# Weighting the values with full-width TensorE blocks instead of two 64-column halves

## The reference

```
scores = where(causal, -1e9, (q @ k.T) / sqrt(D));  scores -= scores.max(-1)
a      = exp(scores);  a /= a.sum(-1) + 1e-9
local  = a @ v
phi(x) = where(x > 0, x, exp(x) - 1) + 1
mem    = (phi(q) @ M_prev) / (phi(q) @ z_prev + 1e-6)
out    = g * mem + (1 - g) * local,   g = sigmoid(beta)
x      = out laid out as (B*S, H*D)
x      = (s * relu(x @ w_in)**2 + b) @ w_out                  # first layer
x      = layernorm(h * softmax(h)) * g_ln @ w_out2, h = x @ w_in2   # second
```

## Time and profile before

| | |
|---|---|
| median of 3 runs | 835.33 us |
| profiled execution | 835.52 us, span 833.5 us |
| PE, PEld busy | 98%, 86% of the span |
| DVE, ACT, POOL busy | 62%, 41%, 41% |
| L662 PE passes, 128 x 64 stationary, 65 moving columns | 1600, 70.9 us busy, mean 226 ns |
| L662 weight loads | 1600, 61.7 us busy, mean 137 ns |
| granted clock of TensorE (mean) | 0.999 |

### The profile page before, as it was taken

The page is one execution under the profiler, slowest core; times in us unless marked ns, Lnnn a source line. Parts: engine busy times, 40 slices in busy tenths (PEclk is TensorE's granted clock), DMA queues, the critical chain, the costliest instruction groups (busy, mean ns, idle before and its releaser), DMA issues.

```text
span 833.5 us, 14412 instructions
## 1 busy us (share of the span) xinstructions
PE 820.2 (98%) x5550; PEld 714.7 (86%) x5550; DVE 513.0 (62%) x1051; ACT 339.4 (41%) x607; POOL 341.3 (41%) x453
## 2 busy tenths in 40 slices
PE   8999999999999999999999999999999999999998
PEld 7788888888878888888888889999998888888886
DVE  8776767667568755333533344345777977777762
ACT  6666666666422223222322232233345434334431
POOL 6666665767599980000000000003368844433300
PEclk9999999999999999999999999999999999999999
DMA  8676767674323330000000000000102000000001
GB/s 148 138 158 140 171 139 172 140 167 103 94 76 103 113 107 7 1 1 0 1 1 1 0 1 1 1 1 1 52 26 75 26 26 23 16 25 26 22 18 50
DMA packets 86370, 49.43 MB, mean 59 GB/s; under 512 B 65056, under 2 KB 73248, under 8 KB 86304
## 3 DMA queue, kind: packets, MB, share of 16 engines
q1 hardware_dynamic: 83760, 47.94, 23.8%
q10 hardware_dynamic: 2544, 0.59, 0.4%
HBM read 27.28 MB, written 4.72 MB: 38 GB/s over the span
## 4 chain that ended last, share of the span: by engine, by line
PE 85%; ACT 6%; DVE 5%; issue 3%; POOL 1%; ACTq 0%; POOLq 0%
PE ps_h L1263 8%; PE ps_h L1265 8%; PE ps_y L1280 8%; PE ps_y L1279 8%; PE ps_h L1264 8%; PE ps_y L1278 8%; PE ps_r L1732 4%; PE ps_r L1730 4%; PE ps_r L1731 4%; PE ps_hid L1667 3%; PE ps_hid L1665 3%; PE ps_hid L1666 3%; PE ps_v L662 3%; PE ps_s L575 3%; ACT pT L792 2%
## 5 line engine op out<-in xcount | busy, mean ns | idle before, releaser
L1380 DVE TENSOR_TENSOR xT<-xT 128x512 f32<-128x512 f32 (+1 forms) x80 | 60.9, 761 | 125.9 <-ACT xT L1338 125.8
L1564 POOL TENSOR_TENSOR win<-stage,win 128x512 fp32r<-128x512 f32 x2 | 2.6, 1294 | 281.6 <-ACT win L1799 281.6
L1280 PE MATMUL ps_y<-g_hi,wout 128*128 128x512 f32 (+1 forms) x320 | 117.5, 367 | 0.0
L1279 PE MATMUL ps_y<-g_lo,wout 128*128 128x512 f32 (+1 forms) x320 | 117.5, 367 | 0.0
L1278 PE MATMUL ps_y<-g_hi,wout 128*128 128x512 f32 (+1 forms) x320 | 117.5, 367 | 0.0
L1344 ACT ACTIVATE g_hi<-xT 128x512 fp32r<-128x512 f32 (+1 forms) x80 | 47.2, 590 | 138.4 <-DVE xT L1382 138.4
L1263 PE MATMUL ps_h<-x_hi,win 128*128 128x512 f32 (+1 forms) x280 | 103.0, 368 | 0.4 <-POOL win L1228 0.4
L1265 PE MATMUL ps_h<-x_hi,win 128*128 128x512 f32 (+1 forms) x280 | 102.8, 367 | 0.0
L1264 PE MATMUL ps_h<-x_lo,win 128*128 128x512 f32 (+1 forms) x280 | 102.8, 367 | 0.0
L1338 ACT ACTIVATE xT<-ps_h 128x512 f32<-128x512 f32 (+1 forms) x80 | 44.1, 552 | 136.6 <-PE ps_h L1265 136.5
L1385 DVE TENSOR_TENSOR g_lo<-xT,g_hi 128x512 fp32r<-128x512 f32 (+1 forms) x80 | 66.3, 829 | 52.5 <-ACT g_hi L1344 52.5
(11 more groups left out here) (212 smaller groups left out, 1808.5 us busy)
## 6 DMA issues: line engine op xcount, KB each, us to landing
stacked<-cut SPq DMA_DIRECT2D x56, 288.0 KB, 4.9
out<-res SPq DMA_DIRECT2D x18, 256.0 KB, 2.0
v_raw<-in_v SPq DMA_DIRECT2D x32, 128.0 KB, 2.7
stage<-in_moe_w_in SPq DMA_DIRECT2D x16, 256.0 KB, 2.8
stage<-in_moe_w_out SPq DMA_DIRECT2D x16, 256.0 KB, 2.6
k_raw<-in_k SPq DMA_DIRECT2D x28, 128.0 KB, 2.7
q_raw<-in_q SPq DMA_DIRECT2D x28, 128.0 KB, 3.6
stage<-in_moe_w_in SPq DMA_DIRECT2D x4, 512.0 KB, 3.5
```

Source lines behind the costliest of these rows:

```text
L1279: pe.matmul(out, wout[:, f, HI, w], g_lo[:, r, 0:n], start=False, stop=False)
L1280: ins = pe.matmul(out, wout[:, f, LO, w], g_hi[:, r, 0:n], start=False, stop=(f == FT - 1))
L1380: dve.tensor_tensor(r, r, r, ALU.mult).then_inc(square_done, 1)
```

## The change

`weigh_values` no longer splits a block of rows: one matmul with all its rows (128, or 64 for t = 4) as stationary columns, without a `tile_position`. `warm_up` has 4 full matmuls instead of 10, and ahead of them four with 64 stationary columns at column places 0 and 64, and two with 64 rows of the array (rows 0 to 63 and 64 to 127).

```diff
-    WARM, WARM_BETWEEN = 10, 5
+    WARM, WARM_BETWEEN = 4, 5
...
         def warm_up():
+            for half in (MINE[0], MINE[1], MINE[0], MINE[1]):
+                pe.matmul(ps_s[half, 0:P], ident[:, half], ident[:, :], start=True, stop=True,
+                          tile_position=(0, half.start))
+            for half, at in ((MINE[0], 0), (MINE[1], 512)):
+                pe.matmul(ps_s[:, at:at + P], ident[half, :], ident[half, :], start=True, stop=True,
+                          tile_position=(half.start, 0))
             for _ in range(WARM):
                 pe.matmul(ps_s[:, 0:P], ident[:, :], ident[:, :], start=True, stop=True)
...
             for t in ts:
                 for j in range(t + 1):
-                    at = p_at[j] + P * (t - j)
-                    for half in MINE if rows_of[t] == P else MINE[:1]:
-                        ins = pe.matmul(ps_v[half, par, E1 * t:E1 * (t + 1)],
-                                        pT[par][:, at + half.start:at + half.stop],
-                                        v_raw[h // 2 % 3][:, j, par, :], start=(t == 0), stop=(j == t),
-                                        skip_group_check=True, tile_position=(0, half.start))
+                    at, m = p_at[j] + P * (t - j), rows_of[t]
+                    ins = pe.matmul(ps_v[0:m, par, E1 * t:E1 * (t + 1)], pT[par][:, at:at + m],
+                                    v_raw[h // 2 % 3][:, j, par, :], start=(t == 0),
+                                    stop=(j == t), skip_group_check=True)
```

## The result

| | before | after |
|---|---|---|
| median | 835.42 us (4 runs, 835.31 to 835.7) | 850.86 us (4 runs, 849.7 to 850.91) |
| profiled execution | 835.52, span 833.5 | 850.15, span 847.8 |
| one pair of heads, steady (us) | 13.51 | 14.37 |

The change made the kernel slower by 15.4 us: ratio 1.0181, 95% interval 1.0164 to 1.0199. The forecast was slower by 6.7, so the sign was right, and the time lies above the range.

What follows compares the result with a forecast made beforehand. PE was taken as nearly the bound, tied with the loop through ScalarE and VectorE. Warm-up -0.1, early heads -0.4, ten pairs +5.1, last waiting burst +0.2, late +1.7, tail +0.2: +6.7, 842.2 us; range 838.0 to 844.8.

Steps and rivals of the forecast that it cites:

- the pass: In L662, a full-width fp32 pass takes 0.11 us, set by its weight load, against 0.058 per half-width step.
- the switch: Around each old L662 burst, changing the tiling mode drains TensorE: 0.14 us in and 0.15 to 0.21 out.
- Entry and exit: Gaps at the start and end of an old L662 burst: 0.14 us in, 0.15 to 0.21 out.
- The waits: PE waits at three spots, all in the odd step: 0.50 us in each 13.51 us pair of heads.
- (0,1,2) with what follows it: L662 burst of tiles 0 to 2 plus L575 x3: from 1.60 to 1.86 us, +0.26.
- (3,4) with L607: L662 burst of tiles 3 and 4 plus the transpose behind it: from 1.45 to 1.52 us, +0.07.
- unpositioned 64-row work as free of the entry and the exit: Assumption read from L641 and L642: 64-row matmuls without a position, as at t = 4, show no switching gap.
- the 64-row blocks still switch: Rival: switching remains inside each (3,4) burst, 0.29 us more at 19 places on the chain, 847.7 us; chance 0.03.
- wait (a): Odd-step L662 burst waits for t_loc: 0.22 us more than the even step, from transposes' end to burst's end.
- waits (b) and (c): Odd step, behind the L662 burst: L575 starts about 0.17 us later and its x3 lasts 0.11 longer than in the even step.
- the -0.60 for two x10 bursts of t = 4 alone: Heads 0 to 2: two bursts of only 64-row blocks each lose 0.30 us of entry and exit.
- The forecast's 0.84: Head 31's 50 passes at the tail, 1.96 us before, take 19 x 0.052 - 0.15 = 0.84 us longer.

Runs made afterwards that it cites:

- half the moving columns: Full-width blocks with the old warm-up, value columns 0 to 31 left out of L662 (33 moving columns instead of 65): 852.13 us in one run.
- crossing chunk in fp32: Kernel before, with the 64-row chunk of the crossing (L641 and L642) read as plain fp32 instead of fp32r: 844.05 us in one run.
- one burst a head: Kernel before, halves kept, with one L662 burst per head instead of two from head 3 on: 829.1 us, ratio 0.9917.
- last tile made wide: Full-width blocks with the old warm-up, the t = 4 blocks also given 128 stationary columns: 856.74 us, ratio 1.0249 to the kernel before.
- warm-up only: Kernel before with the new warm-up alone, blocks left in halves: 836.48 us, ratio 1.0006.
- blocks only: The changed kernel with the old warm-up, so only the full-width value blocks differ from the kernel before: 849.7 us, ratio 1.0164.

## Why the prediction was right and where it failed

**Right: the direction, the pass, the switch.** Full-width passes are 0.112 us apart, and the weight load sets that step, shown by after and by half the moving columns. Entry and exit came back with their sizes in after, in the crossing chunk in fp32, and in the 0.60 per pair of one burst a head. The waits stood where they were said to. Two terms of the sum can be measured against each other:

- (0,1,2) with what follows it: 1.29 + 0.58 = 1.87 behind the output transposes, and 1.33 + 0.57 = 1.90 behind the query ones, against 0.85 + 0.75 = 1.60; the ends of single passes over all steady pairs, up to the first L575, give 1.58 against 1.28: **+0.30**. Forecast 1.86, +0.26. The 1.86 was right; the 1.60 was read from a late burst, and the steady ones take 1.57 (118.56 + 0.71 = 119.27 on PE's timeline to 120.05 + 0.79 = 120.84).
- (3,4) with L607: 1.56 + 0.26 = 1.82 against 1.19 + 0.26 = 1.45: **+0.37**. Forecast 1.52, +0.07.

**The step that failed** is the sentence "so I take unpositioned 64-row work as free of the entry and the exit". It was read off L641 and L642, the nearest rows by shape, which are fp32r; the fp32 blocks of t = 4 pay 0.15 in and 0.15 out. The removed `tile_position` did not take the switch away: it moved from the start of the burst to the edge between its 8 full and its 10 narrow passes, and only last tile made wide, which has no narrow pass, is without it. The rival "the 64-row blocks still switch" was the right mechanism, and its 0.03 the wrong chance: one row stood for a whole class, and the row printed the shape but not the number format.

**The path held.** The forecast followed one loop: PE to the key transposes, ScalarE's rounding, VectorE's K, rl and `t_loc`, and back to the odd burst. It let the even (3,4) burst hide in wait (a). After keeps both. From the end of the key transposes to that of `t_loc` it is 3.55 us in both kernels (121.94 to 125.49; 126.26 + 0.71 = 126.97 to 130.52), the load behind it comes 0.12 later in both, and the 0.37 of the even (3,4) burst just fills the 0.39 that this load idled. By the starts in PE's timelines, as means of ten pairs:

| leg of the loop | before | after | longer by | forecast |
|---|---|---|---|---|
| odd (0,1,2) burst to L566 | 2.32 | 2.46 | 0.14 | 0.18 with the last leg |
| L566, odd (3,4) burst, to `cross(h, 0)` | 3.03 | 3.40 | 0.37 | 0.07 |
| even (0,1,2) burst, to the key transposes | 3.75 | 4.06 | 0.31 | 0.26 |
| key transposes to the next odd burst | 4.41 | 4.45 | 0.04 | see above |

The sum is 0.86 where 0.51 was forecast, and 0.30 of the 0.35 between them is the switch in the odd (3,4) burst. Counting PE's work instead gives nearly the same: 2 x (0.30 + 0.37) = 1.34, less the 0.50 of waits, 0.84. That the two counts agree is chance: it takes an added piece that just fills wait (a). In last tile made wide, with another 0.50 of work, the loop has slack and the work alone counts.

The rival that added 0.29 at 19 places came to 847.7. For the ten pairs it gives 5.1 + 2.9 = 8.0, near the 8.6 measured; most of what it lacks lies at the start and at the end of attention.

**By stretch.** Ten pairs: 8.6 where 5.1 was forecast, 3.0 of it the switch and 0.5 the even (0,1,2) bursts. Late: 5 x 0.30 + 6 x 0.37 = 3.7, less the 0.28 of waits (b) and (c) behind the burst at 193.18; 3.4 was measured, 1.9 forecast. Start: the -0.60 for two x10 bursts of t = 4 alone falls away, since they are exactly the narrow passes that still switch. By the starts of the bursts, after is behind by 0.15 at the first (24.48 and 24.63; the clock, below), by 0.32 at the (0,1,2) burst (51.66 and 51.98), by 0.64 at the (3,4) burst (54.33 and 54.97) and by 0.77 at the first steady one. So the (0,1,2) burst gives 0.32 for a forecast of 0.26, and the (3,4) one 0.13 that the forecast did not count. End: +1.2 for a forecast of 0.2; the bursts of heads 30 and 31 switch inside as well. In before PE waited twice here, 0.83 for POOL's `xq` (the row below) and 0.41 for `win`; in after both waits are gone. PE's timeline of before, then of after:

```profile
231.66 0.77 PE L496 MATMUL ps_t<-ident,xq 128*128 128x128 f32 x5 [0.83 <-POOL xq L421]
```

```profile
245.55 3.17 PE L666 MATMUL ps_v<-v_raw,pT 128*128 128x65 f32 x30
248.66 0.50 PE L1266 MATMUL ps_h<-x_hi,win 128*128 128x512 f32 x1
```

The earlier trace rows had 1.96 for the same 25 blocks; of the 1.21 more, 19 x 0.054 = 1.03 are the steps and 0.14 a switch inside. The forecast's 0.84 had no switch inside, and took off an entry that lies before that row begins. From the start of that burst to L1263 it is 0.74 more (2.37 and 3.11), forecast 0.2; the other 0.47 came in before it, where the forecast had head 30's bursts hidden under POOL's chain. The perceptrons' 0.4 us weren't taken apart.

**The warm-up** gained nothing, as forecast; that it lost about 1 us in most executions, as the runs above suggest, was named only as a risk. In after its twenty passes ended at 5.43 where 6.20 ended them before, and the first transposes waited for the keys.

```profile
1.57 1.12 PE L510 MATMUL ps_s<-ident 128*64 128x128 f32 x8 [1.57 <-POOL ident L335]
...
3.36 2.07 PE L516 MATMUL ps_s<-ident 128*128 128x128 f32 x8
5.75 1.33 PE L496 MATMUL ps_v<-ident,pT 128*128 128x128 f32 x5 [0.32 <-DMA pT<-in_k]
```

## What to carry to other kernels

Two half-width tiles side by side are worth their switches when the weight load sets the pace: a pair takes 0.058 us where one full-width pass takes 0.112, and a burst pays 0.29 once. A block of 128 rows is two such steps and saves 0.108, so by these sizes a burst wins from about three blocks on, and the way to save more is to have fewer, longer bursts. A cost read from the nearest row can mislead when the row has the same shape but another number format. And when the added work of an engine comes near the waits that another loop leaves it, price the loop and the work both: here they tied within 0.04 us, and with 0.5 us more a pair the work alone counted.

## What the runs showed of the hardware

- A plain fp32 matmul with 64 stationary columns pays the switch with or without a given position: in crossing chunk in fp32, 0.20 us from the pass before to its first pass and 0.29 for the full-width piece behind it. The same shape in fp32r takes 0.03, with 0.17 behind it. The Trainium skill, TensorEngine Tiling (Array Packing), section Tiling Modes, ties the drain to a change of mode; the 64-column blocks without a position behave as if they changed it, and the fp32r ones as if they did not. Why the formats differ no run here shows.
- TensorE's pace does not double at a fixed time, even with the same warm-up. In the kernel before the twenty passes took 4.63 us; in last tile made wide the same twenty took 3.88, and the transposes behind them were at full pace at once (0.77 for five). With the new warm-up on the kernel before, two groups of five still ran at half pace, the 1.2 GHz level, 1.3 us each (PE's timelines of last tile made wide, then of warm-up only):

```profile
1.57 3.88 PE L510 MATMUL ps_s<-ident 128*128 128x128 f32 x20 [1.57 <-POOL ident L335]
6.00 0.77 PE L496 MATMUL ps_v<-ident,pT 128*128 128x128 f32 x5 [0.55 <-DMA pT<-in_k]
```

```profile
5.90 1.33 PE L496 MATMUL ps_v<-ident,pT 128*128 128x128 f32 x5 [0.47 <-DMA pT<-in_k]
7.02 1.27 PE L504 MATMUL ps_x<-ident,pT 128*128 128x128 f32 x5
```

The first burst of `weigh_values` moves with it, from 24.31 in last tile made wide to 25.57 in warm-up only (24.48 in before), so one profile of each can't rank the warm-ups.

- The clock can also fall where PE hardly waits. In half the moving columns it was granted at 0.51 for 7 us at the end of attention, with PE busy for 5.74 of the 6 us before and all through it (windows view). At half the clock some 3.4 us of those 7 are lost, more than the 2.4 by which that run lies above blocks only:

```profile
240.00:246.00 6.00, 5.74 (x52) 5.24 (x50) 3.70 (x5) 4.36 (x9) 4.92 (x8) 1.00 0.01 3
246.00:253.00 7.00, 7.00 (x31) 6.10 (x31) 1.21 (x3) 0.00 (x0) 5.23 (x6) 0.51 0.25 75
```
